# Expert weights on one Trainium2 core: bounds read once, one of eight weight splits on GpSimd, the second row copy on ScalarE

## The chip, the cores and the metric

The kernel runs on one core of a Trainium2 chip. The metric is device time in microseconds (us), the median of several runs. TensorE multiplies, VectorE, ScalarE and GpSimd work elementwise, SyncE starts transfers; all of them run side by side and are ordered by semaphores.

## The reference

Chunked attention is followed by a dense layer and by a mixture of eight experts, of which each token uses one or none. The change touches the experts alone:

```python
skip_score = x @ w_skip
do_compute = skip_score > 0
out = x.copy()
xc = x[do_compute]                      # x: 4608 x 512
logits = xc @ w_gate                    # 8 experts
e_idx = np.argmax(logits, axis=1)
gate_w = ...                            # softmax probability of the expert taken
for e in range(8):
    mask = e_idx == e
    h = np.maximum(xc[mask] @ w1[e], 0.0)            # w1[e]: 512 x 1024
    y[mask] = gate_w[mask, None] * (h @ w2[e])       # w2[e]: 1024 x 512
out[do_compute] = xc + y
```

## The kernel before, in words

Every matrix product is made of three: each operand is split into a rounded part ("hi", made by ScalarE) and the remainder ("lo", made by VectorE as original minus hi), and TensorE adds lo x hi, hi x lo and hi x hi.

Up to about 945 us the kernel computes attention and the dense layer. Then come the experts. Tokens have been sorted to experts through a table in memory; each expert takes its tokens in tiles of 128 rows. In this run there are 30 tiles, numbered k = 0 to 29. Experts 0 and 1 have two tiles each (k = 0 and 2, k = 1 and 3), experts 2 and 3 one, 4 and 5 two, expert 6 many, expert 7 the last ones.

The weights of an expert are 128 x 8192 numbers, in eight jobs (EXPERT_JOBS) of 128 x 1024. For experts 2 to 7, ScalarE's split2 makes hi of a job and VectorE's split2 then makes lo of it; both are written into the first tile of the expert before (`more`), spread between the tile's other operations. Such a tile is called a split tile here: k = 3, 4, 5, 6, 8 and 10. The raw data of a job are loaded again, for the expert after that, once VectorE has split it: load_behind on ScalarE waits for raw2_done and issues the transfer, LAG = 3 jobs behind its own split; LATE = 1 of them (job 7) is issued in the next split tile, behind its first hi of h.

A tile k goes like this on TensorE (expert_tile, L871): turn_h(k, 0) transposes the first half of h; up(par, 1) computes the second half; turn_rows(k + 1) transposes the next tile's rows; down, first half, waits for hl_done (VectorE's lo_of_h(k, 0)); turn_h(k, 1); first_half(k + 1) starts the next tile and, in a split tile, waits for jobs 0 and 1 of the next expert; down, second half, waits for lo_of_h(k, 1). ScalarE does hi_of_h, relu2 and hi_of_x for these. VectorE does lo_of_h(k, 0), lo_of_x(k + 1), stage_rows(k + 1), lo_of_h(k, 1), finish(k) and take_rows(k + 1). GpSimd gathers rows for tile k + 2 (gather, which waits for the row numbers in idx) and scatters the finished ones (scatter, which waits for finish).

stage_rows (L1337) copies the gathered rows x_rows to x_next, the row numbers to next_held, and then the next row numbers into idx; take_rows moves x_next to x_held for the addition at the end.

Which tiles belong to an expert is known only at run time: VectorE computes a row `bounds` in tile 0. Each engine reads (value_load) the two bounds of an expert ahead of its first tile. Experts 2 to 5 are two passes of a loop over pairs, so that there the place of the bounds is itself computed:

```python
with dve.Fori(1, E // 2 - 1) as pair:
    expert(pair * 2, 1, True)
    expert(pair * 2 + 1, 0, True)
```

Of the kernel before, what the change touches and what calls it, by code (L numbers as in the profile page):

```python
# [5 lines left out]
ALU = mybir.AluOpType  # L6
ACT = mybir.ActivationFunctionType
AX = mybir.AxisListType
F32 = mybir.dt.float32
# [8 lines left out]
def chunked_attention_moe(nc, first_qk_rows, first_v_rows, qk, v, w_in, w_out, moe_s, moe_b, gate_rows, gate_cols_in, w1, w2, out):  # L18
# [53 lines left out]
    with ctx:  # L72
        def sb(name, shape, dt):
            return ctx.enter_context(nc.sbuf_tensor(name, shape, dt))
# [4 lines left out]
        def sem(name):  # L79
            return ctx.enter_context(nc.semaphore(name))  # L80
# [48 lines left out]
        tiles_i = sb("tiles_i", [1, E], I32)  # L129
        tiles_f = sb("tiles_f", [1, E], F32)  # L130
        gate_cols = sb("gate_cols", [P, KT, E + 1], F32)
        bounds_f = sb("bounds_f", [1, 2 * E + 3], F32)

        bounds = sb("bounds", [1, 2 * E + 3], I32)
        got = sb("got", [P, 2], I32)


# [145 lines left out]
        raw2_in = [sem(f"raw2_in{n}") for n in range(EXPERT_JOBS)]  # L283
        hi2_split = sem("hi2_split")
        raw2_done = sem("raw2_done")
        got_in = sem("got_in")
        first_closed = sem("first_closed")
        x_blank = sem("x_blank")
        next_ready = sem("next_ready")
        rows_in = sem("rows_in")  # L290
        rows_held = sem("rows_held")
        rows_taken = sem("rows_taken")
# [224 lines left out]
        def _(pool):  # L517
# [40 lines left out]
            def send_records(i):  # L558

                pool.wait_ge(table_clear, 16)  # L560
                pool.wait_ge(records_ready, i + 1)
                for t in range(SUB):
                    pool.indirect_dma_start(
                        out=table[:, :], out_offset=bass.IndirectOffsetOnAxis(ap=slot[:, t:t + 1].bitcast(U32), axis=0),
                        in_=record[:, t, :], in_offset=None, bounds_check=E * REGION - 1,
                        oob_is_err=False).then_inc(records_out, 16)
# [58 lines left out]
                    in_=y_rows, in_offset=None, bounds_check=N - 1, oob_is_err=False).then_inc(y_free, 16)  # L625


            send_records(TILES - 2)
            pool.wait_ge(dots_done, DOTS * (TILES - 1))
            pool.memset(x_rows, 0.0).then_inc(x_blank, 1)  # L630
# [5 lines left out]
            send_records(TILES - 1)  # L636
            pool.wait_ge(bounds_ready, 1)
            last = pool.value_load(bounds[0:1, E + 2:E + 3], min_val=64, max_val=16 * (N // P + E + 2))
            with pool.Fori(48, last, 16) as count:
                gather(count, TILES)  # L640
                scatter(count)
            scatter(last)


# [1 line left out]
        def _(pe):  # L646
# [174 lines left out]
            def weights_by(e, jobs):  # L821

                if soon(e):
                    pe.wait_ge(soon_done[e], jobs)
                else:
                    pe.wait_ge(raw2_done, (e - SOON) * EXPERT_JOBS + jobs)

            def up(par, f, part=range(KT)):

# [78 lines left out]
            pe.wait_ge(bounds_ready, 1)  # L908

            def expert(e, par, more):  # L910
                lo = pe.value_load(bounds[0:1, bass.ds(e, 1)], min_val=0, max_val=N // P + E)
                last = pe.value_load(bounds[0:1, bass.ds(e + E + 3, 1)], min_val=0, max_val=N // P + E)
                with pe.If(last > lo):
                    with pe.Fori(lo, last) as k:
                        expert_tile(k, e, par, par)
                if more:
                    expert_tile(last, e, par, 1 - par, more)
                else:
                    last_tile(last, e, par, 1 - par)

            expert(0, 1, True)
            expert(1, 0, True)
            with pe.Fori(1, E // 2 - 1) as pair:
                expert(pair * 2, 1, True)
                expert(pair * 2 + 1, 0, True)
            expert(E - 2, 1, True)
            expert(E - 1, 0, False)


        @block.scalar  # L930
        def _(act):
# [118 lines left out]
            def hi_of_x(k):  # L1050
                act.wait_ge(rows_turned, k + 1)
                keep(XH.rearrange("p k n -> p (k n)"), t_ps[:, :]).then_inc(xh_done, 1)

            def relu2(k, f):
                act.wait_ge(eh_done, 2 * k + f + 1)
                act.activation(h_rows, h_ps[f][:, :], ACT.Relu).then_inc(relu_done, 1)
# [5 lines left out]
            def expert_tile(k, e, par, more, reload, late=False):  # L1062

                def split_next(jobs):
                    for j in jobs if more else ():
                        split2(e + 1, 1 - par, j)
                        if reload and j >= LAG:
                            load_behind(e + 2, j - LAG)

                hi_of_h(k, 0)  # L1070
                for j in range(EXPERT_JOBS - LATE, EXPERT_JOBS) if late else ():
                    load_behind(e + 1, j)
                split_next((0, 1))
                relu2(k, 1)
                hi_of_x(k + 1)
                split_next((2, 3, 4))
                hi_of_h(k, 1)
                split_next((5, 6))
                relu2(k + 1, 0)
                split_next((7,))  # L1080
                for j in range(EXPERT_JOBS - LAG, EXPERT_JOBS - LATE) if reload else ():
                    load_behind(e + 2, j)

            LAG = 3
            LATE = 1

            def load_behind(e, j):
                act.wait_ge(raw2_done, (e - SOON - 1) * EXPERT_JOBS + j + 1)
                load_weights(nc.scalar, e, j)

            hi_of_x(0)
# [7 lines left out]
            hi_of_h(0, 0)  # L1099
            relu2(0, 1)  # L1100
            hi_of_x(1)
            split2(1, 0, EXPERT_JOBS - 2)
            hi_of_h(0, 1)
            split2(1, 0, EXPERT_JOBS - 1)
# [1 line left out]
            expert_tile(1, 1, 0, False, False)  # L1106
            act.wait_ge(bounds_ready, 1)

            def expert(e, par, more, reload, late):
                lo = act.value_load(bounds[0:1, bass.ds(e, 1)], min_val=0, max_val=N // P + E)  # L1110
                hi = act.value_load(bounds[0:1, bass.ds(e + 1, 1)], min_val=1, max_val=N // P + E)
                expert_tile(lo, e, par, more, reload, late)
                with act.If(hi > lo + 1):
                    with act.Fori(lo + 1, hi) as k:
                        expert_tile(k, e, par, False, False)

            expert(0, 1, False, False, False)
            expert(1, 0, True, True, False)
            with act.Fori(1, E // 2 - 1) as pair:
                expert(pair * 2, 1, True, True, True)  # L1120
                expert(pair * 2 + 1, 0, True, True, True)
            expert(E - 2, 1, True, False, True)
            expert(E - 1, 0, False, False, False)


        @block.vector
        def _(dve):
# [208 lines left out]

            def stage_rows(k):  # L1337

                dve.wait_ge(rows_in, 16 * k + 16)
                if not (isinstance(k, int) and k == 1):  # L1340
                    dve.wait_ge(rows_taken, k)
                dve.tensor_copy(x_next, x_rows)
                dve.tensor_copy(next_held[:, :], idx[:, :]).then_inc(next_ready, 1)
                if not (isinstance(k, int) and k == 1):
                    dve.wait_ge(next_ready, k)
                    next_records(k + 1)

            def take_rows(k):
# [15 lines left out]
            def expert_tile(k, e, par, more):  # L1364
                def split_next(jobs):
                    for j in jobs if more else ():
                        split2(e + 1, 1 - par, j)

                lo_of_h(k, 0)
                split_next((0, 1))  # L1370
                lo_of_x(k + 1)
                stage_rows(k + 1)
                split_next((2, 3))
                lo_of_h(k, 1)
                split_next((4, 5, 6, 7))
                finish(k)
                take_rows(k + 1)
# [29 lines left out]
            step(7 + E, dve.tensor_scalar(bounds_f[:, 1:2], bounds_f[:, 1:2], 1.0, None, ALU.add))  # L1407
            step(8 + E, dve.tensor_scalar(bounds_f[:, E + 1:E + 2], bounds_f[:, E:E + 1], 16.0, 16.0, ALU.mult, ALU.add))
            step(9 + E, dve.tensor_scalar(bounds_f[:, E + 2:E + 3], bounds_f[:, E:E + 1], 16.0, 32.0, ALU.mult, ALU.add))
            step(10 + E, dve.tensor_scalar(bounds_f[:, E + 3:], bounds_f[:, 1:E + 1], -1.0, None, ALU.add))  # L1410
            dve.tensor_copy(bounds[:, :], bounds_f[:, :]).then_inc(bounds_ready, 1)
            lo_of_x(1)
            stage_rows(1)
            split2(1, 0, EXPERT_JOBS - 2)
            lo_of_h(0, 1)
            dve.wait_ge(next_ready, 1)
            next_records(2)
            split2(1, 0, EXPERT_JOBS - 1)
            finish(0)
            take_rows(1)  # L1420
            expert_tile(1, 1, 0, False)

            def expert(e, par, more):
                lo = dve.value_load(bounds[0:1, bass.ds(e, 1)], min_val=0, max_val=N // P + E)
                hi = dve.value_load(bounds[0:1, bass.ds(e + 1, 1)], min_val=1, max_val=N // P + E)
                expert_tile(lo, e, par, more)
                with dve.If(hi > lo + 1):
                    with dve.Fori(lo + 1, hi) as k:
                        expert_tile(k, e, par, False)

            expert(0, 1, False)
            expert(1, 0, True)
            with dve.Fori(1, E // 2 - 1) as pair:
                expert(pair * 2, 1, True)
                expert(pair * 2 + 1, 0, True)
            expert(E - 2, 1, True)
            expert(E - 1, 0, False)


def lay_out(inputs):  # L1440
# [57 lines left out]
```

## Time and profile before

| | us |
|---|---|
| median of 3 runs | 1342.43 |
| lowest, highest | 1341.69, 1343.39 |
| profiled execution, own time | 1340.88 |
| its span in the trace | 1339.1 |
| TensorE matmul busy | 1324.7 (99%) |
| VectorE busy | 929.5 (69%) |
| ScalarE busy | 753.7 (56%) |
| GpSimd busy | 311.0 (23%) |

The span runs from the first to the last instruction; the execution's own time is 1.8 us longer. Matmuls overlap each other in the trace, so busy time of TensorE says little about its pace; the starts of its instructions tell it. Times in the rows below are microseconds from the start of the span.

### The profile page before, as it was taken

The numbers are of one execution on the slowest core, as the hardware profiler recorded it, in microseconds if no ns is written. First come the engines' busy times: TensorE is split into PE (matmuls) and PEld (weight loads), VectorE is DVE, ScalarE is ACT, GpSimd is POOL, SyncE is SP. The second block draws the span as 40 slices with busy tenths as digits, with TensorE's granted clock in tenths as the row PEclk, the third lists the DMA queues.
The fourth block names the chain that finished last, engine by engine and source line by source line (L and its number), as shares of the span: only waits on it lengthen the run. The fifth ranks groups of instructions, "written<-read, shape, count | busy, mean of one in ns | idle before, by whom it ended". The sixth has DMA issues, their size and how long they took to land.

```text
span 1339.1 us, 21173 instructions
## 1 busy us (share of the span) xinstructions
PE 1324.7 (99%) x7066; PEld 1168.6 (87%) x7067; DVE 929.5 (69%) x2141; ACT 753.7 (56%) x1838; POOL 311.0 (23%) x274
## 2 busy tenths in 40 slices
PE   8999999999999999999999999999998999999999
PEld 7998999999999999999999999988777778888887
DVE  4877879688787968788797878867648673333332
ACT  4885757576675757566665766746446552222222
POOL 5642222221322212121322222101111111111111
PEclk9999999999999999999999999999999999999999
DMA  7431303031120303122130303044618641111110
GB/s 280 166 121 46 99 29 99 21 106 37 42 97 28 103 28 97 34 69 70 33 106 21 106 25 97 18 142 111 245 55 299 229 143 47 39 47 40 44 42 27
DMA packets 61577, 116.77 MB, mean 87 GB/s; under 512 B 11849, under 2 KB 20297, under 8 KB 61361
## 3 DMA queue, kind: packets, MB, share of 16 engines
q1 hardware_dynamic: 44496, 81.11, 18.5%
q10 hardware_dynamic: 10880, 20.97, 4.5%
q0 software_dynamic: 6112, 13.56, 3.2%
q8 instruction: 49, 0.80, 0.2%
q14 instruction: 40, 0.32, 0.1%
HBM read 91.28 MB, written 27.08 MB: 88 GB/s over the span
## 4 chain that ended last, share of the span: by engine, by line
PE 90%; DVE 5%; issue 2%; ACT 1%; DMA 1%; DVEq 1%; SPq 0%; ACTq 0%
PE h_ps L722 29%; PE y_ps L737 29%; PE y_ps L846 11%; PE h_ps L832 10%; PE s_ps L687 3%; PE av_ps L703 3%; DVE weights_lo L1196 2%; PE t_ps L694 1%; PE s_ps L840 1%; PE t_ps L818 1%; PE av_ps L840 1%; DMA first_raw<-in_first_qk 1%; DVE rows_t_lo L1328 0%; DVE weights_lo L1187 0%; DVE g_lo L1202 0%
## 5 line engine op out<-in xcount | busy, mean ns | idle before, releaser
L1223 DVE CUSTOM_DVE_ANT_0 products<-scratch,wide 128x512 f32<-128x512 f32 x297 | 287.5, 968 | 8.1 <-DVE logits L1223 0.5
L722 PE MATMUL h_ps<-rows_t_hi,weights_lo 128*128 128x384 f32 (+2 forms) x776 | 261.8, 337 | 0.5 <-DVE rows_t_lo L1181 0.5
L722 PE MATMUL h_ps<-rows_t_hi,weights_hi 128*128 128x384 f32 (+2 forms) x776 | 261.1, 336 | 0.0
L722 PE MATMUL h_ps<-rows_t_lo,weights_hi 128*128 128x384 f32 (+2 forms) x776 | 259.9, 335 | 0.0
L1002 ACT ACTIVATE scratch<-h_ps 128x384 f32<-128x384 f32 x192 | 94.5, 492 | 283.6 <-PE h_ps L722 281.7
L737 PE MATMUL y_ps<-weights_hi,g_lo 128*128 128x512 f32 x576 | 228.0, 396 | 1.6 <-DVE g_lo L1202 1.5
L737 PE MATMUL y_ps<-weights_lo,g_hi 128*128 128x512 f32 x576 | 226.4, 393 | 0.0
L737 PE MATMUL y_ps<-weights_hi,g_hi 128*128 128x512 f32 x576 | 225.9, 392 | 0.0
L1202 DVE TENSOR_TENSOR g_lo<-scratch,g_hi 128x384 fp32r<-128x384 f32 x192 | 120.2, 626 | 83.2 <-ACT g_hi L933 80.3
L722 PEld LDWEIGHTS h_ps<-rows_t_hi,weights_lo 128*128 128x128 f32 x776 | 145.8, 188 | 12.7 <-DVE rows_t_lo L1156 4.5
L544 POOL TENSOR_TENSOR qk_lo<-qk_raw,qk_hi 128x768 fp32r<-128x768 f32 x66 | 125.2, 1897 | 135.4 <-ACT qk_hi L933 135.4
L722 PEld LDWEIGHTS h_ps<-rows_t_lo,weights_hi 128*128 128x128 f32 x776 | 145.7, 188 | 7.2
L550 POOL TENSOR_TENSOR v_lo<-v_raw,v_hi 128x256 fp32r<-128x256 f32 x66 | 49.1, 744 | 436.4 <-ACT v_hi L933 436.4
L722 PEld LDWEIGHTS h_ps<-rows_t_hi,weights_hi 128*128 128x128 f32 x776 | 145.6, 188 | 0.0
L737 PEld LDWEIGHTS y_ps<-weights_hi,g_hi 128*128 128x128 f32 x576 | 108.1, 188 | 23.7
L737 PEld LDWEIGHTS y_ps<-weights_hi,g_lo 128*128 128x128 f32 x576 | 108.2, 188 | 20.6 <-DVE g_lo L1202 2.7
L737 PEld LDWEIGHTS y_ps<-weights_lo,g_hi 128*128 128x128 f32 x576 | 108.2, 188 | 17.0 <-issue 0.2
L950 ACT ACTIVATE soft<-s_ps,row_bias 64x64 f32<-64x64 f32 x528 | 120.5, 303 | 3.0
L933 ACT ACTIVATE rows_t_hi<-av_ps 64x256 fp32r<-64x256 f32 (+2 forms) x165 | 68.2, 413 | 64.6 <-PE av_ps L840 56.7
L933 ACT ACTIVATE g_hi<-scratch 128x384 fp32r<-128x384 f32 x192 | 100.8, 525 | 6.3
L846 PE MATMUL y_ps<-weights_hi,rows_t_lo 128*128 128x512 f32 x240 | 97.3, 406 | 6.0 <-DVE rows_t_lo L1328 5.7
L1006 ACT ACTIVATE scratch<-scratch 128x384 f32<-128x384 f32 x192 | 99.6, 519 | 3.7
(178 smaller groups left out, 2372.3 us busy)
## 6 DMA issues: line engine op xcount, KB each, us to landing
qk_raw<-in_qk SPq DMA_DIRECT2D x66, 384.0 KB, 3.0
expert_raw<-in_w ACTq DMA_DIRECT2D x25, 512.0 KB, 5.4
expert_raw<-in_w SPq DMA_DIRECT2D x21, 512.0 KB, 5.7
out<-scratch SPq DMA_DIRECT2D x12, 768.0 KB
x_rows<-scratch SPq DMA_DIRECT2D x12, 768.0 KB
v_raw<-in_v SPq DMA_DIRECT2D x66, 128.0 KB, 2.0
scratch<-in_w ACTq DMA_DIRECT2D x15, 512.0 KB
wide<-in_w_out SPq DMA_DIRECT2D x7, 512.0 KB, 4.8
```

Of the source, the lines that this page charges most:

```text
L544: pool.tensor_tensor(qk_rest[:, :], qk_raw[:, c % SLOTS, :], qk_top[:, :].bitcast(F32), ALU.subtract).then_inc(qk_split, 1)
L550: pool.tensor_tensor(v_lo[:, :], v_raw[:, :], v_hi[:, :].bitcast(F32), ALU.subtract).then_inc(v_split, 1)
L722: mm = pe.matmul(h_ps[f % 2][:, begin:end], w[:, f // PAIR, kt, fs], x[:, z, kt, begin:end], start=kt == 0 and n == 0, stop=kt == KT - 1 a ...
L737: mm = pe.matmul(y_ps[t][:, :], g[:, f % 2, ts], w[:, f, :], start=f == 0 and n == 0, stop=f == FT - 1 and n == 2)
L832: mm = pe.matmul(h_ps[f][:, :], x[:, kt, :], w[par][:, f, kt, :], start=kt == 0 and n == 0, stop=kt == KT - 1 and n == 2)
L846: mm = pe.matmul(y_ps[0][:, :], h[:, t, :], w[par][:, t, :], start=t == 0 and n == 0, stop=t == ET - 1 and n == 2)
L933: return act.activation(out_, in_, ACT.Copy)
L950: last = act.activation(probs[xs, c % 2, h, :], s_blocks[xs, h, x, :], ACT.Exp, bias=row_bias[xs, h:h + 1], scale=SCALE)
L1002: act.activation(r_buf[f % 2], h_ps[f % 2][:, 0:TOK], ACT.Relu).then_inc(r_done, 1)
L1006: act.activation(u_buf[f % 2], r_buf[f % 2], ACT.Square).then_inc(u_done, 1)
L1202: dve.tensor_tensor(GL[:, f % 2, :], u_buf[f % 2], GH[:, f % 2, :].bitcast(F32), ALU.subtract).then_inc(g_ready, 1)
L1223: dve.tensor_tensor_reduce(products[:, :], x2_sb[:, t, :], gate_w[:, e, :], 1.0, 0.0, ALU.mult, ALU.add, logits[:, t, e:e + 1]).then_inc(d ...
```

## The change

Pairs of experts are no loop any more: every engine has the eight experts written out. ScalarE and VectorE read all nine bounds in a row, ahead of tile 2, and keep them in registers. TensorE still reads two for each expert. GpSimd has a loop for each expert, whose ends come from nine more numbers in `bounds`.

For experts 2 to 7, lo of job 0 is made by GpSimd (split_first), ahead of its loop over the tiles of the expert before, behind the scatter of that expert's predecessor. TensorE and the load of job 0 wait for raw2_first.

The copy of x_rows to x_next is made by ScalarE (copy_next), behind hi_of_x; VectorE waits for next_copied before it copies the next row numbers.

LATE is 3: the loads of jobs 5, 6 and 7 are issued in the tile in which they are split, behind ScalarE's first hi of h.

```diff
+            def split_first(e, par):
+                pool.wait_ge(hi2_split, (e - SOON) * EXPERT_JOBS + 1)
+                pool.tensor_tensor(WL[par][:, 0:STAGE], raw_place(e, 0), WH[par][:, 0:STAGE].bitcast(F32),
+                                   ALU.subtract).then_inc(raw2_first, 1)
...
-            with pool.Fori(48, last, 16) as count:
-                gather(count, TILES)
-                scatter(count)
+            begin = 48
+            for e in range(E - 1):
+                if e + 1 > SOON - 1 and e > 0:
+                    split_first(e + 1, 1 - (e + 1) % 2)
+                end = last
+                if e < E - 2:
+                    end = pool.value_load(bounds[0:1, 2 * E + 4 + e:2 * E + 5 + e], min_val=64, max_val=16 * (N // P + E + 3))
+                with pool.Fori(begin, end, 16) as count:
+                    gather(count, TILES)
+                    scatter(count)
+                begin = end
...
-                    pe.wait_ge(raw2_done, (e - SOON) * EXPERT_JOBS + jobs)
+                    pe.wait_ge(raw2_first, e - SOON + 1)
+                    pe.wait_ge(raw2_done, (e - SOON) * (EXPERT_JOBS - 1) + jobs - 1)
...
+            def copy_next(k):
+                if not (isinstance(k, int) and k == 1):
+                    act.wait_ge(rows_taken, k)
+                keep(x_next, x_rows).then_inc(next_copied, 1)
...
                 hi_of_x(k + 1)
+                copy_next(k + 1)
                 split_next((2, 3, 4))
...
-            LATE = 1
+            LATE = 3
             def load_behind(e, j):
-                act.wait_ge(raw2_done, (e - SOON - 1) * EXPERT_JOBS + j + 1)
+                if j == 0:
+                    act.wait_ge(raw2_first, e - SOON)
+                else:
+                    act.wait_ge(raw2_done, (e - SOON - 1) * (EXPERT_JOBS - 1) + j)
                 load_weights(nc.scalar, e, j)
...
+            ends = [act.value_load(bounds[0:1, e:e + 1], min_val=2, max_val=N // P + E) for e in range(E + 1)]
...
             def stage_rows(k):
-                dve.wait_ge(rows_in, 16 * k + 16)
                 if not (isinstance(k, int) and k == 1):
                     dve.wait_ge(rows_taken, k)
-                dve.tensor_copy(x_next, x_rows)
                 dve.tensor_copy(next_held[:, :], idx[:, :]).then_inc(next_ready, 1)
                 if not (isinstance(k, int) and k == 1):
                     dve.wait_ge(next_ready, k)
+                    dve.wait_ge(next_copied, k)
                     next_records(k + 1)
...
-                split_next((0, 1))
+                split_next((1,))
...
+            step(11 + E, dve.tensor_scalar(bounds_f[:, 2 * E + 3:], bounds_f[:, 0:E + 1], 16.0, 48.0, ALU.mult, ALU.add))
...
+            dve.wait_ge(bounds_ready, 1)
+            ends = [dve.value_load(bounds[0:1, e:e + 1], min_val=2, max_val=N // P + E) for e in range(E + 1)]
             def expert(e, par, more):
-                lo = dve.value_load(bounds[0:1, bass.ds(e, 1)], min_val=0, max_val=N // P + E)
-                hi = dve.value_load(bounds[0:1, bass.ds(e + 1, 1)], min_val=1, max_val=N // P + E)
+                lo, hi = ends[e], ends[e + 1]
...
+            for e in range(E):
+                expert(e, 1 - e % 2, SOON <= e + 1 < E)
```

## Rows read from the trace of the kernel before

**Rows 1.** Timeline of TensorE: the first transposes of tiles (start us, us, operation).

```profile
981.36 0.60 PE L840 MATMUL s_ps<-ident,wide 128*128 128x128 f32 x4
...
993.85 0.60 PE L840 MATMUL s_ps<-ident,wide 128*128 128x128 f32 x4
...
1007.08 0.60 PE L840 MATMUL s_ps<-ident,wide 128*128 128x128 f32 x4
...
1051.24 0.60 PE L840 MATMUL s_ps<-ident,wide 128*128 128x128 f32 x4
...
1063.80 0.60 PE L840 MATMUL s_ps<-ident,wide 128*128 128x128 f32 x4
...
1076.73 0.60 PE L840 MATMUL s_ps<-ident,wide 128*128 128x128 f32 x4
...
1114.84 0.60 PE L840 MATMUL s_ps<-ident,wide 128*128 128x128 f32 x4
...
1324.53 0.60 PE L840 MATMUL s_ps<-ident,wide 128*128 128x128 f32 x4
```

**Rows 2.** Chain of waits in a tile without splits (start us, us, what).

```profile
1127.76 2.77 PE h_ps L832 x12
```

**Rows 3.** Windows: a split tile (length, busy us, PEclk, DMA share, GB/s).

```profile
1009.00:1023.50 14.50, 12.81 (x62) 10.06 (x61) 12.77 (x19) 10.45 (x13) 2.20 (x2) 1.00 0.85 289
```

**Rows 4.** Timeline of VectorE: first h splits, weight splits, copy ([idle before <- releaser]).

```profile
984.15 0.69 DVE L1328 TENSOR_TENSOR rows_t_lo<-s_ps,rows_t_hi 128x512 fp32r<-128x512 f32 x1 [1.17 <-issue]
...
1011.48 0.69 DVE L1328 TENSOR_TENSOR rows_t_lo<-s_ps,rows_t_hi 128x512 fp32r<-128x512 f32 x1 [1.42 <-issue]
1012.08 2.35 DVE L1196 TENSOR_TENSOR weights_lo<-expert_raw,weights_hi 128x1024 fp32r<-128x1024 f32 x2
...
1014.95 0.42 DVE L1342 COPY wide<-wide 128x512 f32<-128x512 f32 x1
...
1054.07 0.69 DVE L1328 TENSOR_TENSOR rows_t_lo<-s_ps,rows_t_hi 128x512 fp32r<-128x512 f32 x1
```

**Rows 5.** Timeline of TensorE: the first down product of tile 2.

```profile
985.09 0.49 PE L846 MATMUL y_ps<-weights_hi,rows_t_lo 128*128 128x512 f32 x1
```

**Rows 6.** By line, GpSimd's splits (ns min/median/max, first and last start us).

```profile
L550 POOL TENSOR_TENSOR v_lo<-v_raw,v_hi x66: 737/737/939, 45.6 to 869.4; 128x256 fp32r<-128x256 f32 x66
L544 POOL TENSOR_TENSOR qk_lo<-qk_raw,qk_hi x66: 1832/1850/2170, 31.8 to 851.2; 128x768 fp32r<-128x768 f32 x66
```

**Rows 7.** GpSimd and VectorE at 126 us, and two lines of VectorE.

```profile
126.16 1.85 POOL L544 TENSOR_TENSOR qk_lo<-qk_raw,qk_hi 128x768 fp32r<-128x768 f32 x1 [0.97 <-ACT qk_hi L933]
...
126.22 2.35 DVE L1223 CUSTOM_DVE_ANT_0 products<-scratch,wide 128x512 f32<-128x512 f32 x1
...
L1223 DVE CUSTOM_DVE_ANT_0 products<-scratch,wide x297: 677/692/2347, 110.4 to 914.7; 128x512 f32<-128x512 f32 x149
...
L1134 DVE TENSOR_TENSOR probs_t_lo<-t_ps,probs_t_hi x132: 416/422/428, 45.2 to 869.6; 64x256 fp32r<-64x256 f32 x132
```

**Rows 8.** Timeline of ScalarE: an issue, two weight splits, a first hi of h.

```profile
1009.82 0.40 ACTq L364 DMA_DIRECT2D expert_raw<-in_w  x1
...
1010.35 2.00 ACT L933 ACTIVATE weights_hi<-expert_raw 128x1024 fp32r<-128x1024 f32 x2 [0.16 <-issue]
...
1064.43 0.60 ACT L933 ACTIVATE rows_t_hi<-s_ps 128x512 fp32r<-128x512 f32 x1 [2.56 <-PE s_ps L840]
```

**Rows 9.** Timeline: VectorE's finish and the scatter behind it on GpSimd.

```profile
1064.06 0.75 DVE L1361 SCALAR_TENSOR_TENSOR wide<-y_ps,held,wide 128x512 f32<-128x512 f32 x1 [4.17 <-PE y_ps L846]
...
1065.68 1.00 POOL L623 DMA_INDIRECT out<-wide,sent  x1 [6.51 <-DVE wide L1361]
```

**Rows 10.** TensorE ahead of the clock's fall, and the window behind it.

```profile
948.39 2.82 PE L898 MATMUL s_ps<-gate_cols,scratch 128*128 128x9 f32 x24 [0.90 <-ACT scratch L933]
...
951.50:954.90 3.40, 3.40 (x14) 2.30 (x13) 3.02 (x14) 0.22 (x1) 0.00 (x0) 0.50 0.72 255
```

**Rows 11.** DMA issues (KB each, median us to landing).

```profile
expert_raw<-in_w ACTq DMA_DIRECT2D x25, 512.0 KB, 5.4
```

More of the change, by code:

```diff
@@ L131, in chunked_attention_moe @@
         gate_cols = sb("gate_cols", [P, KT, E + 1], F32)
-        bounds_f = sb("bounds_f", [1, 2 * E + 3], F32)
-        bounds = sb("bounds", [1, 2 * E + 3], I32)
+        bounds_f = sb("bounds_f", [1, 3 * E + 4], F32)
+        bounds = sb("bounds", [1, 3 * E + 4], I32)
         got = sb("got", [P, 2], I32)
@@ L285, in chunked_attention_moe @@
         raw2_done = sem("raw2_done")
+        raw2_first = sem("raw2_first")
         got_in = sem("got_in")
@@ L289, in chunked_attention_moe @@
         next_ready = sem("next_ready")
+        next_copied = sem("next_copied")
         rows_in = sem("rows_in")
@@ L910, in expert @@
             def expert(e, par, more):
-                lo = pe.value_load(bounds[0:1, bass.ds(e, 1)], min_val=0, max_val=N // P + E)
-                last = pe.value_load(bounds[0:1, bass.ds(e + E + 3, 1)], min_val=0, max_val=N // P + E)
+                lo = pe.value_load(bounds[0:1, e:e + 1], min_val=0, max_val=N // P + E)
+                last = pe.value_load(bounds[0:1, e + E + 3:e + E + 4], min_val=0, max_val=N // P + E)
                 with pe.If(last > lo):
@@ L919, in expert @@
                     last_tile(last, e, par, 1 - par)
[L921 to L927, printed above, removed]
+            for e in range(E):
+                expert(e, 1 - e % 2, e < E - 1)
         @block.scalar
@@ L1101, in _ @@
             hi_of_x(1)
+            copy_next(1)
             split2(1, 0, EXPERT_JOBS - 2)
@@ L1107, in _ @@
             act.wait_ge(bounds_ready, 1)
+            ends = [act.value_load(bounds[0:1, e:e + 1], min_val=2, max_val=N // P + E) for e in range(E + 1)]
             def expert(e, par, more, reload, late):
-                lo = act.value_load(bounds[0:1, bass.ds(e, 1)], min_val=0, max_val=N // P + E)
-                hi = act.value_load(bounds[0:1, bass.ds(e + 1, 1)], min_val=1, max_val=N // P + E)
+                lo, hi = ends[e], ends[e + 1]
                 expert_tile(lo, e, par, more, reload, late)
@@ L1115, in expert @@
                         expert_tile(k, e, par, False, False)
[L1117 to L1123, printed above, removed]
+            for e in range(E):
+                expert(e, 1 - e % 2, SOON <= e + 1 < E, SOON <= e + 1 < E - 1, SOON <= e < E - 1)
         @block.vector
@@ L1409, in _ @@
             step(9 + E, dve.tensor_scalar(bounds_f[:, E + 2:E + 3], bounds_f[:, E:E + 1], 16.0, 32.0, ALU.mult, ALU.add))
-            step(10 + E, dve.tensor_scalar(bounds_f[:, E + 3:], bounds_f[:, 1:E + 1], -1.0, None, ALU.add))
+            step(10 + E, dve.tensor_scalar(bounds_f[:, E + 3:2 * E + 3], bounds_f[:, 1:E + 1], -1.0, None, ALU.add))
+            step(11 + E, dve.tensor_scalar(bounds_f[:, 2 * E + 3:], bounds_f[:, 0:E + 1], 16.0, 48.0, ALU.mult, ALU.add))
             dve.tensor_copy(bounds[:, :], bounds_f[:, :]).then_inc(bounds_ready, 1)
@@ L1416, in _ @@
             dve.wait_ge(next_ready, 1)
+            dve.wait_ge(next_copied, 1)
             next_records(2)
@@ L1421, in _ @@
             expert_tile(1, 1, 0, False)
+            dve.wait_ge(bounds_ready, 1)
+            ends = [dve.value_load(bounds[0:1, e:e + 1], min_val=2, max_val=N // P + E) for e in range(E + 1)]
             def expert(e, par, more):
-                lo = dve.value_load(bounds[0:1, bass.ds(e, 1)], min_val=0, max_val=N // P + E)
-                hi = dve.value_load(bounds[0:1, bass.ds(e + 1, 1)], min_val=1, max_val=N // P + E)
+                lo, hi = ends[e], ends[e + 1]
                 expert_tile(lo, e, par, more)
@@ L1429, in expert @@
                         expert_tile(k, e, par, False)
[L1431 to L1437, printed above, removed]
+            for e in range(E):
+                expert(e, 1 - e % 2, SOON <= e + 1 < E)
 def lay_out(inputs):
```

## The prediction

> **What bounds the kernel now.** I read three views. First, when TensorE starts the first transpose of each expert tile [rows 1]: from 1114.84 us it does so every 12.33 us ((1324.53 - 1114.84)/17), and the chain of waits [rows 2] fills that with TensorE alone: four runs of twelve products at 2.77 (11.1), the rest three sets of transposes. That is the floor of a tile; nothing on another engine can be seen in it. While weights of the next expert are split the floor isn't kept: 44.16 us for the three tiles from 1007.08 to 1051.24 (14.72 each), 12.93 for the lone one from 1063.80 to 1076.73. Ten tiles, 981.36 to 1114.84, take 133.48 us against 123.3 at the floor, so 10.2 us is all that the edits on the expert tiles can win.
>
> Second, the windows [rows 3]: from 1009.0 to 1023.5 VectorE is busy 12.77 of 14.50 us, more than the floor. Third, VectorE in order of time [rows 4]: such a tile is one unbroken string: eight splits at a pitch of about 1.14 (two back to back take 2.35 and overlap the next), five row operations, the x_next copy, and ahead of the tile 1.42 us without work, in which it reads the bounds of a new expert. Its first h split so comes late, and the products that need it wait. So VectorE sets the length of these tiles, TensorE that of all others.
>
> **What each part costs.** Zero is the start of a tile's first transpose; the floor's chain puts turn_rows at 3.2, down at 3.6, the second transposes at 6.4, first_half at 6.8, the second down at 9.6.
>
> *Reads of bounds.* Ahead of the h split at 984.15 VectorE stands for 1.17 us with two reads, ahead of the one at 1011.48 for 1.42 (here the branch back is in it), and a tile with no reads starts at once (1054.07) [rows 4]. So a read is 0.59 to 0.71; I take 0.63. The nine in a row stand ahead of lo_of_h(2, 0), seven more than now: 7 x 0.63 = 4.4 us. Behind them on VectorE is that h split (984.15, then 988.6), and TensorE's down, at 985.09 with nothing to spare [rows 5], moves to 989.5. ScalarE reads nine too, but begins earlier, while TensorE is still in the tile before, and has only to be done ahead of VectorE: hidden by VectorE's reads, and about 1.5 us of its own if those were gone. Price +4.4 once; bounds 2 (reads overlap each other) and 5.0. In each later expert the reads taken away are 1.4 to 1.5 us of VectorE's string. Reads on TensorE and GpSimd lie in their queues' slack, as they do now.
>
> *The x_next copy.* VectorE loses 0.33 a tile (its 0.42 [rows 4], less about 0.1 that rows of VectorE overlap their followers), ScalarE gains about 0.5, a 128x512 operation of 0.60 [rows 8] less such an overlap. VectorE's new wait, next_copied, has the record copy, all later splits and GpSimd's gather behind it. ScalarE makes this copy right behind its rounding of the turned rows, while VectorE does lo_of_x and a small copy, 0.7 together: 0. In tiles without splits both engines wait for TensorE anyway. If the cover went, each 0.1 would be 0.1 of VectorE's string.
>
> *Split 0 on GpSimd.* VectorE loses 1.14. GpSimd took 1.85 for 768 columns and 0.74 for 256 [rows 6], so 0.74 + 3 x 0.56 = 2.4 for 1024; bounds 2.2 to 2.6. But the two engines exclude each other [rows 7]: the product of two SBUF tensors that starts at 126.22, just behind GpSimd's at 126.16, lasts 2.35 instead of 0.69: it does its work when GpSimd ends. The split of a PSUM tensor never rises over 0.428. So GpSimd's 2.4 us shut out VectorE's weight splits, not its splits of turned rows and h. The Trainium skill says the same (GPSIMD Engine Reference, Specifications: SBUF interfaces shared with VectorE, contention when VectorE has two SBUF inputs), and this trace agrees (2.35 against 0.69). That page's 4.5 us for 2048 columns would make an estimate of 2.25 for the split and the sum about 1 us smaller.
>
> *Late loads.* With LATE = 3 three DMA issues, 0.40 each on ScalarE [rows 8], stand ahead of split 0, and the last waits until VectorE has done the previous tile's job 7. Two are gone from the end of the tile before, where they waited for VectorE as well. The 1.2 us lie ahead of both of ScalarE's first splits.
>
> *The strings put together.* A lone split tile (there are two, the first from 1063.80): ScalarE's h row at 0.6, issues to 2.0, split 0 to 3.1, split 1 to 4.1 (two take 2.00 [rows 8]). GpSimd's scatter begins 1.62 after finish does [rows 9] and ends at 2.9, its split runs 3.1 to 5.5. VectorE's split 1, ready at 4.1, ends at 5.5 + 1.1 = 6.6, lo_of_x at 7.25: first_half 0.5 late. Then idx 7.5, splits 2 and 3, the second h at 9.9 to 10.6: the second down another 0.6 late. 12.33 + 1.1 = 13.45, against 12.93 now: +0.5 each, +1.0.
> The three in a row (VectorE comes out of the tile before with 1.4 us of work left over): its finish starts at 1.7, job 7's load goes to 2.3, ScalarE's splits end at 3.35 and 4.3, VectorE's split 1 is first (4.35 to 5.5), GpSimd runs 5.5 to 7.9 (scatter 3.3 to 4.3), and TensorE's first_half needs it: 8.1 instead of 7.0. VectorE's split 2 ends at 9.0, the second h at 10.8, down at 10.9, next tile at 13.6. The same by VectorE's sum: 14.7 - 1.14 - 0.33 - 1.5 = 11.7, plus 0.6 waiting for ScalarE's split 1 and 1.3 shut out at split 2: 13.6. Three times: 40.8 against 44.16, -3.4.
> The first (993.85): GpSimd is ready at 3.1, VectorE at 3.15, a toss: 13.25 or 12.5, I take 12.9 against 13.23: -0.3. The tiles without splits between them stay near 12.6, since their first h split is late in either kernel.
>
> *Clock.* TensorE would stand still for some 4.6 us. The nearest row: after a wait of 0.9 and 24 products of nine columns the granted clock was 0.50 (1.2 GHz) from 951.5 to 954.9 [rows 10], so that 3.4 us did the work of 1.7. Bounds 0 and 1.7; I take 1.3, nearer to that row, since a halt is less work than it shows and some of the slow stretch may fall into the halt. The Trainium skill (TensorE: Matmul & The Clock Gate, Part 1: The HAM clock gate) has an idle TensorE drop to 1.2 GHz, which rows 10 fit.
>
> *The rest.* One bound step more on VectorE (0.2) pushes lo_of_x(1) into about 0.3 us of slack; writing the experts out saves or costs at most what branches take now, which lies in the 1.42 of an expert's start: 0 beside it.
>
> Sum: 4.4 + 1.0 - 3.4 - 0.3 + 1.3 = +3.0. The profiled execution, span 1339.1 and own time 1340.88, becomes 1342.1 and 1343.9; the median lies 1.55 above it: 1345.4.
>
> **Rivals.**
> *Splits reach the floor (faster).* GpSimd's split lies in VectorE's gap before split 1 and shuts out nothing. For it: VectorE's sum of 11.7 is under 12.33. Against it: 2.35 in rows 7. It decides if GpSimd's split starts before about 2.3 and ends under 4.8. Tiles at 12.33 to 12.5: -9, with the halt and clock +5.7: 1339.1, and 1337.7 without the clock's part. Chance 0.2.
> *The halt is short, or the change does next to nothing.* Reads overlap or ScalarE's and TensorE's slack takes them: +2, no fall of the clock; the tiles -2.7: 1341.7. For it: the fixed pair's 1.17 includes work that isn't repeated. Against it: the two reads of a later expert stand for 1.42, no less. Chance 0.14.
> *Loads come late.* Jobs 5 to 7 are issued at 0.8 to 2.3 of the tile that splits them; a load lands after a median of 5.4 us [rows 11], and while the DMA is 0.85 busy [rows 3] I allow 8: 10.3 against ScalarE's split 5 at 9.9 (8.8 in lone tiles, where the DMA is idle). 0.5 to 1 in each of four tiles: +3: 1348.4. Chance 0.1.
>
> **Numbers.** The likeliest is the sum, 0.56, from 1343.5 (clock stays) to 1346.5. A measurement of this kernel tells 0.2% (2.7 us: 1339.7 and 1345.1) from no change. Of the 0.56 about 0.3 lies above 1345.1. Slower 0.3 + 0.1 = 0.40; same 0.26 + 0.14 = 0.40; faster 0.20. Range: without the tenth below 1338.3 (half of the first rival) and the tenth above 1348.5.
>
> **What would show it.** Right: TensorE idle for about 4.4 us before the tile-2 down, VectorE's h split at 988.6 and not 984.15, behind nine reads; GpSimd's six splits near 2.4 us; a VectorE split of 1 or 2 recorded at 2 us or more in each split tile; tiles of 13.6 and 13.45. Wrong: no long VectorE split (then the floor), a halt under 3, ScalarE waiting for a DMA before split 5, or PEclk at 1.00 behind the halt (then 1344.1).

## The result, and the profile after

The changed kernel takes 1352.07 us (median, 1351.78 to 1352.41), the kernel before, beside it, 1342.91: ratio 1.0059, 95% interval 1.004 to 1.0078. It is slower, by 9.2 us. The forecast was 1345.4, and the time lies above its range. The profiled execution has a span of 1350.0 us and an own time of 1352.16, against 1339.1 and 1340.88.

The same timeline as in [rows 1], the first transposes of TensorE (start us, us, operation), now reads:

```profile
983.82 0.60 PE L857 MATMUL s_ps<-ident,wide 128*128 128x128 f32 x4
1003.57 0.60 PE L857 MATMUL s_ps<-ident,wide 128*128 128x128 f32 x4
1016.80 0.60 PE L857 MATMUL s_ps<-ident,wide 128*128 128x128 f32 x4
1031.37 0.60 PE L857 MATMUL s_ps<-ident,wide 128*128 128x128 f32 x4
...
1060.55 0.60 PE L857 MATMUL s_ps<-ident,wide 128*128 128x128 f32 x4
1073.15 0.60 PE L857 MATMUL s_ps<-ident,wide 128*128 128x128 f32 x4
1086.72 0.60 PE L857 MATMUL s_ps<-ident,wide 128*128 128x128 f32 x4
...
1125.81 0.60 PE L857 MATMUL s_ps<-ident,wide 128*128 128x128 f32 x4
...
1335.41 0.60 PE L857 MATMUL s_ps<-ident,wide 128*128 128x128 f32 x4
```

The ten tiles from 983.82 to 1125.81 take 141.99 us, against 133.48 [rows 1]: +8.5, the same as the 9.2 of the medians within their interval (5.4 to 10.5 us). Seventeen tiles behind them take 209.60 against 209.69: nothing. Tile 2 starts 2.46 us later than before (983.82 against 981.36), and tile 0 already did so (959.10 against 956.63); this arises far ahead of the expert tiles: from 9.4 to 14.8 us TensorE does 24 products in the one profile and 47 in the other. It belongs to the two executions, so the comparison goes by lengths of tiles. Two places lost time.

**Tile 2: 19.75 us instead of 12.49.** VectorE, then TensorE, then the windows of the halt and of what follows (length, busy us of PE, PEld, DVE, ACT, POOL, PEclk, DMA share, GB/s):

```profile
985.28 0.16 DVE L1370 COPY held<-next_held 128x2 int32<-128x2 int32 x1
991.18 0.69 DVE L1346 TENSOR_TENSOR rows_t_lo<-s_ps,rows_t_hi 128x512 fp32r<-128x512 f32 x1 [5.74 <-issue]
```

```profile
992.11 0.79 PE L863 MATMUL y_ps<-weights_hi,rows_t_lo 128*128 128x512 f32 x1 [4.50 <-DVE rows_t_lo L1346]
...
997.40 0.86 PE L857 MATMUL av_ps<-ident,wide 128*128 128x128 f32 x4
```

```profile
983.80:991.10 7.30, 3.81 (x21) 3.00 (x19) 1.25 (x3) 2.12 (x4) 1.00 (x1) 1.00 0.09 35
991.10:997.90 6.80, 5.79 (x15) 4.53 (x16) 1.53 (x4) 0.00 (x0) 1.04 (x1) 0.50 0.06 11
```

VectorE stands for 5.74 us ahead of its h split (1.17 before [rows 4]): the nine reads. TensorE halts for 4.50, and then does the twelve products of down in 5.29 us (992.11 to 997.40) instead of 2.77 [rows 2]: the granted clock is 0.50 there, the 1.2 GHz level, and full speed comes back only at 997.9.

**The split tiles.** The three in a row take 14.57, 14.60 and 14.58 us, 43.75 together (44.16 before, 40.8 forecast), the lone ones 13.57. VectorE, GpSimd and TensorE in tile 4, which starts at 1016.80:

```profile
1019.65 0.69 DVE L1346 TENSOR_TENSOR rows_t_lo<-s_ps,rows_t_hi 128x512 fp32r<-128x512 f32 x1
1020.94 3.61 DVE L1214 TENSOR_TENSOR weights_lo<-expert_raw,weights_hi 128x1024 fp32r<-128x1024 f32 x1 [0.60 <-ACT weights_hi L945]
1024.47 0.68 DVE L1340 TENSOR_TENSOR rows_t_lo<-t_ps,rows_t_hi 128x512 fp32r<-128x512 f32 x1
1025.07 0.15 DVE L1359 COPY next_held<-idx 128x2 int32<-128x2 int32 x1
```

```profile
1020.01 1.01 POOL L625 DMA_INDIRECT out<-wide,sent  x1 [6.96 <-DVE wide L1378]
1021.05 2.41 POOL L633 TENSOR_TENSOR weights_lo<-expert_raw,weights_hi 128x1024 fp32r<-128x1024 f32 x1
```

```profile
1025.20 0.50 PE L849 MATMUL h_ps<-weights_hi,rows_t_lo 128*128 128x512 f32 x1 [1.16 <-DVE rows_t_lo L1340]
...
1028.51 0.50 PE L863 MATMUL y_ps<-weights_hi,rows_t_lo 128*128 128x512 f32 x1 [0.29 <-DVE rows_t_lo L1346]
```

GpSimd's split takes 2.41 us, as forecast. VectorE's split 1 is recorded as starting at 1020.94, 0.11 ahead of it, and lasts 3.61: it ends at 1024.55, 1.09 after GpSimd's end at 1023.46. So it did nearly all of its 1.14 us of work behind GpSimd, though its recorded start is first. lo_of_x stands behind it, and TensorE waits 1.16 us at first_half and 0.29 at the second down.

### The profile page after: what moved, and what is told of

It reads as the page before. It is cut to its first block, busy times and chain, and to the rows that moved or that the text cites. A ratio compares the mean times of both kernels' runs of the same rounds, so it can differ in the third digit from the quotient of the medians.

```text
span 1350.0 us, 21037 instructions
## 1 busy us (share of the span) xinstructions
PE 1330.8 (99%) x7066; PEld 1173.3 (87%) x7066; DVE 922.7 (68%) x2105; ACT 767.4 (57%) x1867; POOL 324.8 (24%) x280
## 4 chain that ended last, share of the span: by engine, by line
PE 89%; DVE 4%; issue 3%; ACT 2%; DMA 1%; DVEq 0%; ACTq 0%; POOL 0%; SPq 0%; POOLq 0%
PE h_ps L738 29%; PE y_ps L753 28%; PE y_ps L863 10%; PE h_ps L849 10%; PE av_ps L719 3%; PE s_ps L703 3%; DVE weights_lo L1214 2%; PE t_ps L710 1%; PE s_ps L857 1%; PE av_ps L857 1%; PE t_ps L834 1%; DMA table<-record,slot 1%; PE h_ps L666 0%; DMA expert_raw<-in_w 0%; ACT rows_t_hi L945 0%
## 5 line engine op out<-in xcount | busy, mean ns | idle before, releaser
L849 PE MATMUL h_ps<-weights_hi,rows_t_lo 128*128 128x512 f32 x244 | 101.9, 417 | 4.4 <-DVE rows_t_lo L1340 4.3
```

What stands on the lines that cost most here:

```text
L849: mm = pe.matmul(h_ps[f][:, :], x[:, kt, :], w[par][:, f, kt, :], start=kt == 0 and n == 0, stop=kt == KT - 1 and n == 2)
```

## The experiments

Each of the eleven kernels below "after" was timed beside the kernel before on the same chip (medians of 1342.99 to 1343.51 us there). The intervals of the ratios are 3 to 9 us wide, so small terms are read from the lengths of tiles, worked out as above; these come from one profile of each kernel, and single tiles of one kernel that should be alike differ by up to 0.6 us in it (j, tiles 4 to 6: 12.64, 13.28, 12.94). t2 is tile 2, t4-6 the three split tiles in a row together, and "ten" counts tiles 7 and 11 too.

```
kernel                    median   ratio to before (95%)    t2     t3     t4-6   t8     t9     t10    ten
before                                                      12.49  13.23  44.16  12.93  12.56  12.95  133.48
after                     1352.07  1.0059 (1.0040, 1.0078)  19.75  13.23  43.75  13.57  12.95  13.57  141.99
b reads in tile 1         1344.93  1.0012 (0.9997, 1.0027)  12.32  13.22  43.82  13.57  12.87  13.57  134.61
c split 0 on VectorE      1342.36  0.9999 (0.9980, 1.0018)  19.77  12.34  37.87  12.59  12.64  12.56  132.96
d one late load           1351.23  1.0055 (1.0035, 1.0075)  19.51  13.25  43.78  13.24  12.85  13.23  140.99
f GpSimd behind split 1   1354.66  1.0089 (1.0057, 1.0121)  19.41  13.07  42.11  14.05  12.84  14.05  140.70
g products in the halt    1349.69  1.0061 (1.0038, 1.0085)  16.97  13.23  43.77  13.57  12.89  14.03  139.61
a reads by expert         1344.82  1.0011 (1.0001, 1.0021)  12.53  13.23  44.10  13.61  12.54  13.57  134.74
h b and c                 1335.52  0.9948 (0.9932, 0.9964)  12.32  12.34  37.84  12.57  12.57  12.56  125.39
i h, one late load        1333.64  0.9926 (0.9913, 0.9939)  12.32  12.34  37.56  12.32  12.34  12.32  124.13
j i, copy on VectorE      1334.24  0.9924 (0.9898, 0.9950)  12.32  12.34  38.85  12.32  12.34  12.32  125.41
k i, reads by expert      1339.24  0.9971 (0.9952, 0.9990)  12.53  12.89  41.54  12.47  12.58  12.43  129.61
l j and k                 1342.00  0.9988 (0.9972, 1.0004)  12.53  13.28  42.81  13.22  12.56  12.81  132.32
```

**b: the reads inside tile 1.** Shown is VectorE's part; ScalarE's nine reads are moved likewise.

```diff
+            lo_of_x(2)
+            stage_rows(2)
+            dve.wait_ge(bounds_ready, 1)
+            read_ends(3)
+            lo_of_h(1, 1)
+            read_ends(6)
+            finish(1)
```

> The changed kernel with the same nine reads of bounds on VectorE and ScalarE, but placed inside tile 1, where both wait for TensorE anyway. My theory: the row of reads ahead of tile 2 costs 4.5 us of halt on TensorE and 2.8 more because its clock then runs at half; both go: tile 2 falls from 19.75 to about 12.5 us, and the whole to about 1344.8, 7.3 below the changed kernel. Rival: the halt of tile 2 is made by something else that comes with the written-out experts (branches, code): then tile 2 stays at 17 us or more, and the whole within 3 us of the changed kernel.

Measured: 7.1 us below the changed kernel, tile 2 at 12.32, the other tiles unchanged; tile 1, which now has the reads in it, takes 12.34 us as in the changed kernel. The rival falls. The six reads now lie in a gap of VectorE in tile 1 that ends at TensorE anyway; 3.08 us stand there without work, and the next tile's h split starts at once:

```profile
980.67 0.69 DVE L1359 TENSOR_TENSOR rows_t_lo<-av_ps,rows_t_hi 128x512 fp32r<-128x512 f32 x1 [2.12 <-ACT rows_t_hi L945]
984.44 0.17 DVE L1389 COPY sent<-held 128x2 int32<-128x2 int32 x1 [3.08 <-issue]
...
986.86 0.69 DVE L1359 TENSOR_TENSOR rows_t_lo<-s_ps,rows_t_hi 128x512 fp32r<-128x512 f32 x1
```

**g: products in the halt**, to part the halt from the clock behind it.

```diff
                 weights_by(e, EXPERT_JOBS)
+                if e == 0 and not isinstance(k, int):
+                    for _ in range(18):
+                        pe.matmul(y_ps[1][:, :], WH[par][:, 0:P], WH[par][:, 0:512], start=True, stop=True)
                 pe.wait_ge(hl_done, 2 * k + 1)
```

> The changed kernel, with 18 products of 512 columns added on TensorE while it waits ahead of tile 2's down; what they write is overwritten and used by nothing. They take 4.2 us, less than the halt. My theory: the halt stays, but the clock stays at 1.00 behind it, and tile 2 takes 16.9 us instead of 19.75: 2.9 us below the changed kernel, which is the price of the clock's fall. Rival: the slow stretch costs less than it seems, since the products are held up by VectorE in it: 1 us or less.

Measured: tile 2 at 16.97, 2.78 less, and the median 2.4 less. TensorE from 987.35, then the window of down behind the products (columns as above):

```profile
987.35 4.38 PE L897 MATMUL y_ps<-weights_hi 128*128 128x512 f32 x18
...
992.01 0.49 PE L863 MATMUL y_ps<-weights_hi,rows_t_lo 128*128 128x512 f32 x1 [0.28 <-DVE rows_t_lo L1349]
```

```profile
992.30:1000.70 8.40, 8.40 (x40) 6.91 (x39) 1.18 (x5) 1.20 (x2) 1.04 (x1) 1.00 0.04 9
```

VectorE's part is as late as before (down at 992.01), the clock stays at 1.00, and 2.8 us are gone. So of the 7.3 us in tile 2 the reads cost 4.5 and the clock 2.8.

**c: split 0 back on VectorE.** GpSimd's split_first is taken out with it.

```diff
-                                  ALU.subtract).then_inc(soon_done[e] if soon(e) else raw2_done, 1)
+                                  ALU.subtract).then_inc(soon_done[e] if soon(e) else raw2_done if j else raw2_first, 1)
...
-                split_next((1,))
+                split_next((0, 1))
```

> The changed kernel with split 0 back on VectorE; nothing else of the change undone. My theory: GpSimd's split shuts VectorE's split 1 out even where VectorE began first, so that the row operations come late; without it no VectorE split is recorded over 1.3 us, the three split tiles in a row (tiles 4 to 6) take 12.9 each instead of 14.6 (5 us in all), the lone ones (8 and 10) about 12.4 instead of 13.6, tile 3 12.4 instead of 13.2: about 8 us below the changed kernel, 1344. Rival: ScalarE with its issues and copy, or VectorE's own sum, sets the string: tiles 4 to 6 stay at 14 or more, and the whole falls by 2 us at most. Second rival: the offload is worth its shutting out (split 0 costs VectorE 1.14 a tile): tiles get longer than 14.6.

Measured: 9.7 us below the changed kernel; tiles 4 to 6 at 12.6 each, tile 3 at 12.34, both rivals far off. VectorE in tile 4, where two splits take 2.36 again:

```profile
1018.72 2.36 DVE L1206 TENSOR_TENSOR weights_lo<-expert_raw,weights_hi 128x1024 fp32r<-128x1024 f32 x2
1021.00 0.69 DVE L1332 TENSOR_TENSOR rows_t_lo<-t_ps,rows_t_hi 128x512 fp32r<-128x512 f32 x1
1021.60 0.16 DVE L1351 COPY next_held<-idx 128x2 int32<-128x2 int32 x1
```

Taking 1.14 us of work off VectorE cost 2 us a tile in a row and about 1 in a lone one. This one edit is worth -9.0 us in the ten tiles (132.96 against 141.99).

**f: GpSimd's split behind VectorE's split 1**, the order that the prediction had assumed.

```diff
-                pool.wait_ge(hi2_split, (e - SOON) * EXPERT_JOBS + 1)
+                pool.wait_ge(raw2_done, (e - SOON) * (EXPERT_JOBS - 1) + 1)
```

> The changed kernel, but GpSimd's split 0 waits until VectorE has done its split 1 of that tile: the order that my prediction assumed for the three tiles in a row. If the order is all that I had wrong, VectorE's splits 1 are 1.2 us or less, splits 2 are the ones recorded at 2.4 to 3.6, the row operations aren't late, and tiles 4 to 6 take 13.6 instead of 14.6: 3 us below the changed kernel. Rival: GpSimd's 2.4 us are lost to VectorE wherever they lie: tiles 4 to 6 stay at 14.4 or more, no change.

Measured: the tiles in a row fall to 14.04, half of what was expected; the lone ones, where GpSimd had had a head start, rise to 14.05. The four times lie far apart (1348.6 to 1358.7), and the rise of their median is not explained: the profile is of the shortest of them, and its ten tiles are 1.3 us shorter than the changed kernel's. The tiles are what this run is read by. Tile 5 starts at 1028.08; VectorE, GpSimd and TensorE in it:

```profile
1028.08 0.60 PE L857 MATMUL s_ps<-ident,wide 128*128 128x128 f32 x4
```

```profile
1033.38 0.69 DVE L1340 TENSOR_TENSOR rows_t_lo<-t_ps,rows_t_hi 128x512 fp32r<-128x512 f32 x1
1033.98 2.00 DVE L1359 COPY next_held<-idx 128x2 int32<-128x2 int32 x1
1036.17 0.17 DVE L1353 COPY idx<-got 128x2 int32<-128x2 int32 x1 [0.20 <-DVE next_held L1359]
1036.25 2.35 DVE L1214 TENSOR_TENSOR weights_lo<-expert_raw,weights_hi 128x1024 fp32r<-128x1024 f32 x2
```

```profile
1033.55 2.40 POOL L633 TENSOR_TENSOR weights_lo<-expert_raw,weights_hi 128x1024 fp32r<-128x1024 f32 x1 [1.25 <-DVE weights_lo L1214]
```

```profile
1036.08 0.49 PE L849 MATMUL h_ps<-weights_hi,rows_t_lo 128*128 128x512 f32 x1 [0.76 <-POOL weights_lo L633]
```

The split of a PSUM tensor runs in GpSimd's time (0.69), as the prediction had it; the copy of 128x2 integers doesn't: 2.00 us instead of 0.15. So of the row operations only lo_of_x fits there, and split 2 starts at 8.17 us of the tile (1036.25) where the prediction had 7.9. The order explains 0.54 us a tile of the miss, the copies about 0.27; the last 0.2 stays open.

**d: one late load.**

```diff
-            LATE = 3
+            LATE = 1
```

> The changed kernel with one load behind the first rounding instead of three (LATE = 1). My theory: two issues of 0.4 us less stand ahead of ScalarE's split 0, so that GpSimd's split starts 0.8 us earlier and ends earlier: the six split tiles shorten by 0.4 to 0.8 each, about 3 us in all. Rival: the two loads at the end of the tile before now wait for VectorE there and delay ScalarE's first relu or h row: no gain, or up to 3 us of loss.

Measured: 0.8 us less, tiles in a row unchanged, the lone ones 0.33 shorter. Both theories miss the size: in a row GpSimd's split was held by the end of its scatter (1020.01 + 1.01 in tile 4, its split at 1021.05), not by ScalarE, so issues ahead of ScalarE's split 0 don't matter.

**a: reads by expert again.**

```diff
-                lo, hi = ends[e], ends[e + 1]
+                lo = dve.value_load(bounds[0:1, e:e + 1], min_val=2, max_val=N // P + E)
+                hi = dve.value_load(bounds[0:1, e + 1:e + 2], min_val=2, max_val=N // P + E)
```

> The changed kernel, with two reads of bounds per expert on VectorE and ScalarE again instead of nine at once; the experts stay written out. My theory: tile 2 goes back to 12.5 us (7.2 less), and each of the three split tiles in a row gets longer by what two reads cost VectorE, 1.2 us each, the lone ones by 0 to 0.5: about 3 us below the changed kernel. Rival: since GpSimd's split is what these tiles end on, VectorE's two reads at their start are hidden behind it: they stay at 14.6, and the whole falls by 7.

Measured: 7.2 us less. The rival was right. VectorE and GpSimd in tile 5:

```profile
1028.36 0.69 DVE L1346 TENSOR_TENSOR rows_t_lo<-s_ps,rows_t_hi 128x512 fp32r<-128x512 f32 x1 [1.09 <-issue]
1028.97 3.08 DVE L1214 TENSOR_TENSOR weights_lo<-expert_raw,weights_hi 128x1024 fp32r<-128x1024 f32 x1
```

```profile
1028.56 2.40 POOL L633 TENSOR_TENSOR weights_lo<-expert_raw,weights_hi 128x1024 fp32r<-128x1024 f32 x1
```

The two reads take 1.09 us, but what follows waits for GpSimd's end at 1030.96 anyway: the time won with the reads was spent standing in front of GpSimd. Against b (134.61) the ten tiles take 134.74: with GpSimd's split in place, reading the bounds once is worth 0.1 us.

**h and i: both repairs, and with them one late load.**

> The changed kernel with both repairs: the nine reads inside tile 1, and split 0 back on VectorE. What is left of the change is the written-out experts with bounds read once, the row copy on ScalarE, and three late loads. My theory: the two costs are separate and add up: tile 2 at 12.3 us, tiles 3 to 11 at 12.4 to 12.6; the whole 16 us below the changed kernel and 7 below the kernel before, about 1336. Rival: the long halt ahead of tile 2 in the run with split 0 on VectorE let ScalarE and the loads get ahead, and hid a wait that now comes back in tiles 3 to 6: 2 to 4 us of the gain go again, about 1339.

> As the one with both repairs, and one late load instead of three. My theory of the string on VectorE: ScalarE's first two splits come 0.8 us earlier, but VectorE, which has no work to spare before them in a split tile, is the one that sets its length: within 1 us of the kernel with both repairs. Rival: the issues at the end of the tile before wait for VectorE's last splits and hold ScalarE's relu and h row back: tiles 4 to 6 over 13 us, 1 to 3 us more. Second rival: ScalarE's splits are what VectorE waits for: up to 1.5 us less.

Measured: 1335.52 and 1333.64, 8.0 and 9.9 us below the kernel before. The two costs add up (141.99 - 7.4 by b - 9.0 by c = 125.6, measured 125.39), and h's rival, a wait hidden by the halt, falls. In i the lone tiles are at the floor, and in tiles 5 and 6 VectorE is one string of 12.64 us without a wait for another engine, 0.3 above it:

```profile
1022.22 0.74 DVE L1383 SCALAR_TENSOR_TENSOR wide<-y_ps,held,wide 128x512 f32<-128x512 f32 x1
...
1024.07 2.35 DVE L1219 TENSOR_TENSOR weights_lo<-expert_raw,weights_hi 128x1024 fp32r<-128x1024 f32 x2
...
1034.86 0.74 DVE L1383 SCALAR_TENSOR_TENSOR wide<-y_ps,held,wide 128x512 f32<-128x512 f32 x1
```

i is the fastest of all: of the 10.2 us between the ten tiles and their floor it takes 9.35.

**j, k, l: the rest of the change, one part at a time taken out of i.** j has the copy on VectorE, k two reads per expert, l both.

```diff
+                dve.wait_ge(rows_in, 16 * k + 16)
                 if not (isinstance(k, int) and k == 1):
                     dve.wait_ge(rows_taken, k)
+                dve.tensor_copy(x_next, x_rows).then_inc(next_copied, 1)
```

> The kernel with both repairs and one late load, but with the x_next copy back on VectorE: what moving that copy is worth by itself. In the kernel with the copy on ScalarE VectorE is one unbroken string of 12.64 us in tiles 5 and 6; the copy adds 0.33 to it: 12.97 in tiles 4 to 6, lone split tiles 12.34 or little more. Together 1 to 1.5 us longer, about 1335. Rival: the move cost ScalarE as much as it saved VectorE: no change.

> The kernel with both repairs and one late load, but with two reads of bounds per expert on VectorE and ScalarE, as the kernel before has them; the copy stays on ScalarE. Each read is 0.61 us of VectorE's string: tiles 4 to 6 at 13.85 instead of 12.6, tile 2 at 12.5, the lone split tiles 12.4 to 12.9: 4 to 5 us longer, about 1338. Rival: with the experts written out the reads cost nothing beside what branches cost: 2 us or less.

> Both undone: two reads per expert, copy on VectorE, split 0 on VectorE, one late load. Of the change only the written-out experts and GpSimd's loops by expert are left. If writing out is worth nothing by itself, as my prediction took it, this is the kernel before again: tiles 4 to 6 at 14.2 to 14.7, 1343 within 1.5. Rival: the branch back and the computed addresses cost VectorE 0.2 us or more an expert: 0.5 to 1.5 us below the kernel before.

Measured by the ten tiles: the copy on ScalarE is worth 1.3 us (j to i; 2.7 from l to k), the early reads 5.5 (k to i). Writing out alone gives 1.2 (132.32 against 133.48), while the medians, 1342.00 against 1342.99 (0.9972 to 1.0004), don't tell it from nothing. For j the medians don't show its 1.3 either (1334.24 and 1333.64); the tiles do. The copy's gain stands on two pairs of profiles that differ in its size, the 1.2 of writing out on one pair, so that it is not shown. The 5.5 is shown by tiles and medians alike (1339.24 against 1333.64), and k's tiles in a row came out at the 13.85 that was expected.

## Why the prediction was wrong

Its steps, in the ten tiles, with what was measured for each:

- *Nine reads ahead of tile 2, +4.4:* 4.50 of halt. Right; without them the halt and the slow clock behind it both go (b).
- *Clock, +1.3:* 2.8 (g). The mechanism was right; the term was mis-sized by half. The slow stretch was 6.8 us and not the 3.4 of [rows 10], and 5.8 of it fell on work. The upper bound of 1.7, from a single row, was too low.
- *Lone tiles, +1.0:* +0.64 and +0.62, nearly right: VectorE's split 1 was recorded at 2.60 behind GpSimd's, as the string had it. Tile 9 between them added 0.39: its first h split comes late out of tile 8 (TensorE waits 0.37 us for it at 1090.90), which the prediction took as equal in either kernel.
- *Three tiles in a row, -3.4:* -0.4. This is the step that failed, and over half of it was the sentence "VectorE's split 1 is first (4.35 to 5.5), GpSimd runs 5.5 to 7.9". The prediction's own numbers didn't bear that order: its scatter ends at 4.3 and its ScalarE split 0 at 3.35, so GpSimd was free at 4.3, 0.05 ahead of VectorE, the same toss that it saw for the first tile. VectorE was first by the record, at 4.14, GpSimd at 4.25, and GpSimd went through. All its 2.4 us then fell on a VectorE that stood still, with lo_of_x behind it, and TensorE waited in first_half. A part of the rest is the idx copies, which the string let run in GpSimd's time: f, with the assumed order, takes 14.04 and not 13.6.
- *Tile 3, -0.3:* 0.0; GpSimd won the toss, as the prediction's 13.25 had it for that case.
- *Copy, late loads, writing out, 0 beside the rest:* the copy is a gain of its own once VectorE is the bound (j). The late loads cost 1.3 us in the ten tiles where nothing else holds (h against i), and at most 1.0 in the changed kernel (d), each from one pair of profiles.

The terms as measured: 4.5 + 2.8 + 1.7 (tiles 8 to 10) - 0.4 + 0.0 = 8.6, against 8.5 by the tiles and 9.2 by the medians; the difference to 3.0 is 1.5 from the clock, 3.0 from the three tiles, and 1.0 from tiles 3 and 8 to 10. Of the rivals, "splits reach the floor" was wrong by 6.8 us in the three tiles in a row alone (43.75 against 37.0) with GpSimd's split and came true to within 0.3 us a tile when it was taken away; "the halt is short" and "loads come late" are excluded by 4.50 and by c and h, where the same late loads hold nobody up by more than 0.3 a tile.

What the prediction missed on a larger scale is that the two halves of the change defeat each other. Without the offload, VectorE's string without reads and copy was 12.6 us (12.9 by the prediction's own sum, 14.7 - 0.33 - 1.5), and that left the offload at most 0.3 us a tile to win, against 2.4 us in which it shuts VectorE out. Each edit was costed only on top of all the others.

## What to carry to other kernels

Cost each part of a change against the bound that the other parts leave behind: an offload is worth at most what the engine still stands above the floor, here 0.3 us a tile. Work put on GpSimd beside a VectorE that splits SBUF tensors can cost VectorE the whole of GpSimd's instruction, here 2.4 us for 1.14 saved, and an order of starts that rests on 0.1 us is not one to build on; cost both orders. Count small SBUF copies as shut out too. Only the split of a PSUM tensor ran beside it (0.69 in f); no run here places GpSimd's split under such work alone, so that this would help is not shown. Work that is done once, as the nine reads, belongs where its engine waits anyway (tile 1), and a halt of TensorE has to be priced with the slow clock behind it.

## What the runs showed of the hardware

- A VectorE split whose recorded start was 0.11 us ahead of GpSimd's was overtaken and lasted 3.61 us (three tiles in a row: 3.61, 3.62, 3.62). The Trainium skill (SBUF — State Buffer, SBUF: two separate sides) gives the pair to whichever starts first, for the whole instruction. That the loser stands for the whole instruction is what the rows show; that the first start wins is not what these recorded starts show. Elsewhere the same lead was enough: in the kernel before, VectorE's split of two SBUF tensors began 0.10 us ahead of GpSimd's, kept its usual 0.56 us, and GpSimd's took 2.16 instead of 1.85 [rows 6]:

```profile
116.04 0.56 DVE L1202 TENSOR_TENSOR g_lo<-scratch,g_hi 128x384 fp32r<-128x384 f32 x1
```

```profile
116.14 2.16 POOL L544 TENSOR_TENSOR qk_lo<-qk_raw,qk_hi 128x768 fp32r<-128x768 f32 x1 [3.41 <-ACT qk_hi L933]
```

  So no lead in recorded starts decides by itself. The two cases differ in what went before: here VectorE's split follows its predecessor at once and GpSimd's comes after 3.41 us without work, while in the tiles in a row VectorE's comes after 0.60 us of waiting and GpSimd's right behind its scatter. Which of these matters stays open, and so does whether VectorE's record begins before it asks for the ports.
- A copy of 128x2 integers from SBUF to SBUF on VectorE, begun 0.43 us behind GpSimd's split, lasted 2.00 us instead of 0.15 and ended with GpSimd's. It has one SBUF source; the Trainium skill (SBUF — State Buffer, Who interferes with whom) counts copies among the operations that can take both port pairs, and this row agrees.
- Reading one bound costs VectorE 0.51 to 0.64 us, and reads don't overlap: six took 3.08 us, nine 5.74, two 1.09.
- After a halt of 4.50 us the granted clock was 0.50 for 6.8 us, 5.8 of them on work; with 4.38 us of unused products in the halt it stayed at 1.00.
